# Attention ahead of two mixture layers: the order of heads in a unit, and of some short steps around it

## Time and profile before

| | |
|---|---|
| time, median of 3 runs | 668.75 us (668.14, 668.75, 670.43) |
| the profiled execution's own time | 668.98 us |
| its span | 667.2 us |
| PE busy | 652.2 us (98%), weight loads 584.9 us (88%) |
| DVE, ACT, POOL busy | 308.9, 303.5, 216.3 us (46%, 45%, 32%) |
| chain that ended last | PE 93%, ACT 3%, DVE 2%, POOL 1% |
| expert products in the chain | inner (L379) 44%, outer (L396) 44% |

### The profile page before, as it was taken

The page is one execution under the profiler, slowest core; times in us unless marked ns, Lnnn a source line. Parts: engine busy times, 40 slices in busy tenths (PEclk is TensorE's granted clock), DMA queues, the critical chain, the costliest instruction groups (busy, mean ns, idle before and its releaser), DMA issues.

```text
span 667.2 us, 9784 instructions
## 1 busy us (share of the span) xinstructions
PE 652.2 (98%) x3716; PEld 584.9 (88%) x3716; DVE 308.9 (46%) x600; ACT 303.5 (45%) x756; POOL 216.3 (32%) x217
## 2 busy tenths in 40 slices
PE   6799999999999999999999999999999999999997
PEld 5678888999999999999999999999999999999996
DVE  7555544212121212121212122215988888889896
ACT  6885555222211222211122211226778787877774
POOL 5666212133310133310133310135632466642221
PEclk9799999999999999999999999999999999999999
DMA  9636300002320001420001320002420000001011
GB/s 318 216 126 234 123 14 1 1 1 63 124 67 1 0 1 52 129 73 1 0 1 42 125 86 1 0 1 64 126 64 1 0 2 1 0 2 48 0 48 48
DMA packets 13079, 36.83 MB, mean 55 GB/s; under 512 B 1832, under 2 KB 2856, under 8 KB 13032
## 3 DMA queue, kind: packets, MB, share of 16 engines
q1 hardware_dynamic: 13032, 36.20, 16.5%
HBM read 33.84 MB, written 2.36 MB: 54 GB/s over the span
## 4 chain that ended last, share of the span: by engine, by line
PE 93%; ACT 3%; DVE 2%; issue 1%; POOL 1%; DMA 0%; POOLq 0%; ACTq 0%; DVEq 0%
PE ps_h L379 44%; PE ps_o L396 44%; ACT scratch L475 1%; PE ps_a L329 1%; PE ps_o L356 1%; PE ps_b L356 1%; DVE scratch L645 1%; PE ps_a L341 0%; DMA scratch<-in_qk_plain 0%; PE ps_a L417 0%; PE ps_q L341 0%; ACT scratch L485 0%; PE ps_h L341 0%; DVE acc L708 0%; POOL scratch L847 0%
## 5 line engine op out<-in xcount | busy, mean ns | idle before, releaser
L379 PE MATMUL ps_h<-x_hi,w_hi 128*128 128x384 f32 (+1 forms) x608 | 201.8, 332 | 1.1 <-POOL w_lo L863 1.1
L379 PE MATMUL ps_h<-x_hi,w_lo 128*128 128x384 f32 (+1 forms) x608 | 199.8, 329 | 0.0
L379 PE MATMUL ps_h<-x_lo,w_hi 128*128 128x384 f32 (+1 forms) x608 | 199.2, 328 | 0.0
L693 DVE SCALAR_TENSOR_TENSOR h_lo<-ps_h,h_hi 128x384 fp32r<-128x384 f32 (+1 forms) x104 | 54.7, 526 | 268.9 <-ACT h_hi L498 268.9
L498 ACT ACTIVATE h_hi<-ps_h 128x384 fp32r<-128x384 f32 (+1 forms) x104 | 48.5, 467 | 285.7 <-PE ps_h L379 285.7
L396 PE MATMUL ps_o<-w_hi,h_lo 128*128 128x512 f32 x432 | 170.8, 395 | 0.0
L396 PE MATMUL ps_o<-w_lo,h_hi 128*128 128x512 f32 x432 | 170.5, 395 | 0.0
L396 PE MATMUL ps_o<-w_hi,h_hi 128*128 128x512 f32 x432 | 169.4, 392 | 1.1 <-POOL w_lo L869 0.6
L863 POOL TENSOR_TENSOR w_lo<-raw,w_hi 128x512 fp32r<-128x512 f32 x48 | 61.8, 1288 | 219.8 <-ACT w_hi L504 219.0
L379 PEld LDWEIGHTS ps_h<-x_hi,w_hi 128*128 128x128 f32 x608 | 114.6, 189 | 8.8 <-issue 1.7
L379 PEld LDWEIGHTS ps_h<-x_lo,w_hi 128*128 128x128 f32 x608 | 114.5, 188 | 5.6
(11 more groups left out here) (80 smaller groups left out, 576.6 us busy)
## 6 DMA issues: line engine op xcount, KB each, us to landing
raw<-in_weights SPq DMA_DIRECT2D x48, 512.0 KB, 3.5
scratch<-in_qk_dil SPq DMA_DIRECT2D x8, 352.0 KB, 4.6
scratch<-in_qk_plain SPq DMA_DIRECT2D x8, 304.0 KB, 5.3
out_t<-acc SPq DMA_DIRECT2D x9, 256.0 KB, 2.1
scratch<-in_v_dil SPq DMA_DIRECT2D x8, 208.0 KB
scratch<-in_v_plain SPq DMA_DIRECT2D x8, 192.0 KB, 4.7
prob<-in_probs SPq DMA_DIRECT2D x1, 18.0 KB, 12.5
a_sb<-in_a SPq DMA_DIRECT2D x1, 2.0 KB, 10.7
```

The lines of the kernel that those rows point to most:

```text
L379: last = nc.tensor.matmul(h_of(k, f), w[:, f, dc, :], x, start=dc == 0 and i == 0, stop=dc == DC - 1 and i == 2)
L693: nc.vector.scalar_tensor_tensor(out=h_lo[:, s % RING, 0:n], in0=h_of(k, f), scalar=0.0, in1=h_hi[:, s % RING, 0:n].bitcast(F32), op0=ALU. ...
```

## The change

- `kind_of` gives 1 for heads 0 to 3 of a unit and 0 for the others. The arrays that the kernel gets are laid out by kind, so a unit now begins with its two dilated pairs and ends with its two plain ones. Masks are zeroed and made in the matching order. As x now has the dilated heads' features first, the rows of w1 of the four experts are put in that order on the host.
- ACT: `exponentials(8)` moves from behind `attention_hi(3)` to ahead of `take_turned(6)`.
- DVE: `invert(8)` moves ahead of `attention_lo(2)`; `invert(9)` moves behind the masks of heads 10 and 11.
- POOL: `normalise(8)` moves ahead of `low_w1(0, 1)`.
- ACT, casts of expert 0: chunk 6 of w1 is cast in slot f = 2 instead of f = 4. In slots f = 4 and 6 the w1 cast goes ahead of the second head's exponentials, and the first w2 cast ahead of `high(k, f + 1)`; the other w2 casts stay at the end.

```diff
-W1_HIGH_AT = ((4,), (5,), (6, 7), ())
+W1_HIGH_AT = ((4,), (5, 6), (7,), ())
 W2_HIGH_AT = ((0, 1), (2,), (3, 4), (5, 6, 7))
...
 def kind_of(head):
-    return 0 if head < PLAIN else 1
+    return 1 if head < PLAIN else 0
...
             high_w1(0, 0)
+            exponentials(HEADS)
             take_turned(6)
             take_turned(7)
             attention_hi(2)
             high_w1(0, 1)
             attention_hi(3)
-            exponentials(HEADS)
             exponentials(HEADS + 1)
...
                     if not (k or f >= LAG):
                         high(k, f + 1)
+                    if k == 0 and f >= LAG:
+                        for c in W1_HIGH_AT[f // 2]:
+                            high_w1(0, c)
                     if more:
                         exponentials(2 * w + 3)
                     attention_hi(w)
+                    if k == 0 and f >= LAG:
+                        high_w2(0, W2_HIGH_AT[f // 2][0])
                     if k or f >= LAG:
                         high(k, f + 1)
-                    if k == 0:
+                    if k == 0 and f < LAG:
                         for c in W1_HIGH_AT[f // 2]:
                             high_w1(0, c)
                         for c in W2_HIGH_AT[f // 2]:
                             high_w2(0, c)
+                    if k == 0 and f >= LAG:
+                        for c in W2_HIGH_AT[f // 2][1:]:
+                            high_w2(0, c)
...
-            for kind, half in ((0, 0), (1, 0), (0, 1), (1, 1)):
+            for kind, half in ((1, 0), (0, 0), (1, 1), (0, 1)):
                 nc.vector.memset(masks[:, kind, half], 0.0).then_inc(masks_zeroed, 1)
...
+            invert(HEADS)
             attention_lo(2)
             attention_lo(3)
-            invert(HEADS)
-            invert(HEADS + 1)
...
                         mask(2 * w + 2)
                         mask(2 * w + 3)
+                    if k == 0 and f == 0:
+                        invert(HEADS + 1)
+                    if more:
                         maximum(2 * w + 2)
                         maximum(2 * w + 3)
...
-                kind, half = n % 2, n // 2
+                kind, half = 1 - n % 2, n // 2
...
             low_w1(0, 0)
+            normalise(HEADS)
             low_w1(0, 1)
-            normalise(HEADS)
             normalise(HEADS + 1)
```

More of the change, by code:

```diff
@@ L820, in make_mask @@
             def make_mask(n):
-                kind, half = n % 2, n // 2
+                kind, half = 1 - n % 2, n // 2
                 tiles = TILES[kind]
-                m = as_tiles(masks[:, kind, half], kind * PLAIN, TQ[kind])
+                m = as_tiles(masks[:, kind, half], (1 - kind) * PLAIN, TQ[kind])
                 pool.wait_ge(masks_zeroed, n + 1)
@@ L971, with chunks @@
         vs.append(vt.transpose(0, 2, 1, 3, 4, 5))
-    def chunks(w_inner, w_outer):
-        wi = w_inner.reshape(DC, P, FC, P).transpose(2, 1, 0, 3).reshape(FC, P, D)
+    def chunks(w_inner, w_outer, order):
+        wi = w_inner.reshape(DC, P, FC, P)[list(order)].transpose(2, 1, 0, 3).reshape(FC, P, D)
         return np.stack([wi, w_outer.reshape(FC, P, D)], axis=2)
-    experts = [chunks(moe_w1[e], moe_w2[e]) for e in range(MOE)]
-    experts += [chunks(moe2_w_in[:, F * i:F * (i + 1)], moe2_w_out[F * i:F * (i + 1)]) for i in range(RATIONAL)]
+    taken = (*range(DC // 2, DC), *range(DC // 2))
+    experts = [chunks(moe_w1[e], moe_w2[e], taken) for e in range(MOE)]
+    experts += [chunks(moe2_w_in[:, F * i:F * (i + 1)], moe2_w_out[F * i:F * (i + 1)], range(DC)) for i in range(RATIONAL)]
     inputs = {
```

## The result

| | before | after |
|---|---|---|
| median | 668.11 us (6 runs, 667.55 to 670.43) | 674.08 us (6 runs, 673.14 to 675.78) |
| ratio, 95% interval | | 1.0087 (1.0068 to 1.0106) |
| own time and span of the profiled execution | 668.98, 667.2 | 675.78, 674.0 |

The change makes the kernel 6 us slower. The forecast was 667.5 and the range ended at 669.6.

What follows compares the result with a forecast made beforehand. PE, nearly always busy behind 70 us, was taken as the bound, so only its entry time could move: +0.1 - 0.6 + 1.0 - 1.9 + 0.2 = -1.2 us, forecast 667.5 against 668.75, range 666.0 to 669.6.

Steps and rivals of the forecast that it cites:

- What is late next: Behind normalise_probs on DVE, masks for turn(8) come late: +0.2 us, bounds 0 to +0.5.
- Stage D: Slots behind f = 0: earlier casts end PE's waits for POOL's low weights, -1.9 us, bounds 1.4 to 2.1 gained.
- Stage A: Head up to values(2) at 20.20: ACT's list with dilated heads first comes to 0.0 us, bounds -0.4 to +0.6.
- Stage B: From 20.20 to turn(4) at 29.00: load slightly later, turn(4) no longer waits for masks; -0.6 us in the sum.
- Stage C: Slot f = 0, turn(4) to turn(5): dilated heads 10 and 11 lengthen the chain, +1.0 us, bounds +0.5 to +1.3.
- R1: PE's clock stays at 2.4 GHz through the pause near 20 us: 666.7 us, chance 0.15.
- R2: Load of w = 5 1 us after 24.4, or head 9 normalised only at 29.3; nothing left: 668.6 us, chance 0.22.
- R3: PE's clock comes back at 33.4 instead of 26.5, so the kernel is slower: 670.2 us, chance 0.08.

Runs made afterwards that it cites:

- e9: Changed kernel with one cast put back, w2 chunk 5 again behind high(0, 7): 667.84 us, ratio 0.9986 to the kernel before.
- e1: Changed kernel with normalise_probs moved on DVE from slot k = 0, f = 6 to the end of slot k = 1, f = 0: 668.19 us.
- e3: Kernel before with dilated heads first and no step moved: 670.26 us, ratio 1.0025 to the kernel before.
- e4: Changed kernel without the addition of 1e-9 to the sums of the probabilities: 674.21 us, ratio 1.0080 to the kernel before.
- e10: Changed kernel without the addition and the multiplication of normalise_probs: 667.91 us, ratio 0.9983 to the kernel before.
- e6: Changed kernel with plain heads first, moved steps kept, normalise_probs at the end of slot k = 1, f = 0: 666.65 us.
- e5: e1 with v of w = 4 and q and k of w = 5 loaded ahead of expert 0's last two weight chunks: 666.41 us.
- e2: Changed kernel with plain heads first again and all moved steps kept: 668.61 us, ratio 0.9997 to the kernel before.

## Why the prediction was wrong

**The step that failed** stands under "What is late next": `normalise_probs` on DVE "ran for 2 us ahead of the `attention_lo`", "I count +0.2; bounds 0 to +0.5". It cost 3.7 us up to `turn(8)`, and 2.9 us more by the clock. I took its 2 us as work of DVE. 1.35 of them were one addition over 9 elements, while a reduction over 36 elements of the same tensors took 0.16; that ratio could be seen in the trace of before, and beside it POOL's two normalisations from 53.99 to 55.61, which the addition outlasted by 0.03. DVE and POOL, before:

```profile
54.09 0.16 DVE L679 TENSOR_REDUCE prob_sum<-prob 128x9 f32<-128x36 f32 x1
54.29 1.35 DVE L681 TENSOR_SCALAR prob_sum<-prob_sum 128x9 f32<-128x9 f32 x1
...
53.99 1.62 POOL L847 TENSOR_TENSOR scratch<-scratch 96x384 f32<-96x384 f32 x2
57.36 3.79 POOL L869 TENSOR_TENSOR w_lo<-raw,w_hi 128x512 fp32r<-128x512 f32 x3 [1.75 <-ACT w_hi L511]
```

So the duration was a wait for POOL's list, and it had to be taken anew once POOL's list moved. And it moved by my own stage D: I followed the earlier casts up to `low_w2(0, 4)` at 50.4, and not to chunks 5 to 7, which could now run behind `normalise(17)` without the pause of 1.75 us that the late casts had left.

**Stage A** was right: 0.0 forecast, -0.06 measured. PE's pause before `values(2)` stayed, 2.03 us for 2.44, the 0.4 less that was forecast. (The 337 GB/s used there is the rate from 3 to 4 us, a window that the earlier trace rows does not show.)

**Stage B** failed too, on the load and on the clock: -0.6 forecast, +1.5 measured at `turn(4)`, and +0.1 to +0.6 in e9, e1, e3, e4 and e10. I put the load at 24.4, bounds up to +1.0 above that. It was 26.1 in the profiled execution of the changed kernel; `scores(5)`, which waited for it, started at about 25.2 in e1, e3, e4 and e10 and at 24.8 in e9. I priced 115 kB at the rates of the earlier trace rows. The rate itself was lower. DMA summaries from 20 to 24 us, before and after:

```profile
DMA packets 1011, 1.37 MB, mean 342 GB/s; under 512 B 392, under 2 KB 639, under 8 KB 1011
```

```profile
DMA packets 757, 1.09 MB, mean 273 GB/s; under 512 B 319, under 2 KB 350, under 8 KB 757
```

0.28 MB less were moved in the same 4 us, which is 1 us at 273 GB/s. It isn't a chance of one execution: the six traces with dilated heads first and the old order of loads have 257 to 284 GB/s there (e3, which changes nothing else, 276), the four with plain heads first 332 to 360. Why packets took longer with the dilated pair's loads in that stretch is open.

The clock is the other part. I let it come back at about 26.5, so that inner (0, 0) would take 1.8 us, from 26.1 to 27.9. It ran from 27.79 to 30.51, all of it at 1.2 GHz, 2.72 us. Of the 2.6 us by which `turn(4)` missed its 27.9, 1.7 are the late start and 0.9 the slow product. The gain of the new order on DVE was there: `turn(4)` no longer waited for masks, and in e6, where PE waits only 0.40 us for the load, the time from `scores(5)` to `turn(4)` is 4.26 us for 4.75, though PE was at 1.2 GHz there until 30.0 (before, 26.6).

**Stage C** was right in kind: +1.0, bounds 0.5 to 1.3, and the wait before `turn(5)` grew to 1.06. From `turn(4)` to `turn(5)` the measured growth is 7.12 - 5.61 = 1.5, in e1 1.4. In e5, where the clock was back before `turn(4)`, it is 6.88 - 5.61 = 1.3, the upper bound, with a wait of 1.34 for the forecast 1.4; the rest in the other two is probably the lower clock, which no run tests by itself.

**Stage D** was right: -1.9 forecast (bounds 1.4 to 2.1), -2.1 measured between `turn(5)` and inner (1, 0), with both waits for POOL gone.

**The rivals.** R1 is out. R2's condition, a load about 1 us later than 24.4, came true, and so did R3's in kind, a clock that comes back late after pauses of PE: at 32.3, 5.7 us later. Both are in the 3.0 us at `turn(5)`, where 0.5 was forecast. But e1, with `turn(5)` 2.0 us late and the clock back at 30.5, is still below the kernel before, so the two don't make the change slower. None of the rivals had the addition. Its price, 6.6 us, is more than the whole loss; without it the change is worth -0.7 (e1), or -1.2 with one cast put back (e9). That e9 meets the -1.2 of the forecast is luck: by inner (1, 0) it has gained 0.6 of the 1.4 that stages A to D were to give, and the rest comes behind, where the sum had nothing.

## What to carry to other kernels

Before a DVE instruction's duration is put in a sum, compare it with its elements: if it takes far longer than its neighbours of the same size, look at POOL's timeline beside it. If it ends when POOL's work ends, its price changes when POOL's list does. In these runs the small fp32 addition and the multiplication with two SBUF inputs belonged in a pause of POOL; reductions, reciprocals and instructions with one input in PSUM kept their durations beside it. When casts are moved earlier, follow the engine behind them to the end of its list: a pause that disappears there may have been what let another engine through.

## What the runs showed of the hardware

- An addition over 9 elements and a multiplication over 36 took 4.66 and 4.37 us beside four GpSimd instructions in a row (changed kernel, e4), and 0.17 and 0.20 us with GpSimd idle. The addition was let in by GpSimd's pauses of 0.79 us (e9) and 0.19 us (e2); the multiplication was let in once between two subtractions without a pause (e2).
- PE's clock fell to 1.2 GHz at 63.0 after PE had worked 1.68 us of the 4 before 62, and was back at 69.8. This cost 2.9 us by the steps from `turn(8)` to inner (1, 1), and 2.9 in e4 as well. In e2, where PE's waits at that place were 0.68 and 0.62 us, the clock stayed at 2.4 GHz.
- The DMA engines moved 276 GB/s instead of 342 from 20 to 24 us (e3 and before), after only the order of pairs of 304 and 352 KB had changed.
